# The last stores of a chunked attention with two mixtures of experts: when they are issued, and when the transposes of absent blocks are let go

## The reference

```
# attention within chunks of 64 tokens; q, k, v are (4, 8, 576, 64)
scores = scale * (q_c @ k_c.T); attn = softmax(scores); out = attn @ v_c
x = out as (N = 2304 tokens, D = 512)

# first mixture: all 4 experts on all tokens, F = 1024
x = sum over e of p[:, e] * (relu(x @ w1[e]) @ w2[e])

# second mixture: each token goes to one of 8 experts
expert_idx = argmax(x @ w_gate); gate_w = softmax(x @ w_gate) at expert_idx
out[mask] = gate_w[mask] * (relu(x[mask] @ w1[e]) @ w2[e])     # mask: tokens of expert e
```

## Time and profile before

| what | value |
|---|---|
| median of three executions | 1142.42 us (1140.51 to 1144.55) |
| the profiled execution | 1139.17 us |
| its span, first to last instruction | 1137.4 us |
| mean granted TensorE clock | 0.993 of full speed |
| TensorE busy | 1114.6 us, 98% of the span |
| VectorE busy | 563.9 us, 50% |
| ScalarE busy | 289.4 us, 25% |
| GpSimd busy | 312.3 us, 27% |
| transposes of hidden rows | 38, median 5.1 us to landing |
| stores to the output | 23 (22 from `rows`, one from the block ahead) |

### The profile page before, as it was taken

The page is one execution under the profiler, slowest core; times in us unless marked ns, Lnnn a source line. Parts: engine busy times, 40 slices in busy tenths (PEclk is TensorE's granted clock), DMA queues, the critical chain, the costliest instruction groups (busy, mean ns, idle before and its releaser), DMA issues.

```text
span 1137.4 us, 19057 instructions
## 1 busy us (share of the span) xinstructions
PE 1114.6 (98%) x6750; PEld 976.2 (86%) x6750; DVE 563.9 (50%) x1142; ACT 289.4 (25%) x429; POOL 312.3 (27%) x191
## 2 busy tenths in 40 slices
PE   9999999999999999999999999999999989999995
PEld 6899888999889999988999998889877778888884
DVE  5445434322221232222223248888655358988985
ACT  3444344331111133111113311112242023032220
POOL 7300000250000024000002401100377759168781
PEclk9999999999999999999999999999999989999998
DMA  9332221420000021000002101101672459379996
GB/s 355 79 103 83 74 74 28 150 74 0 0 0 0 0 82 65 0 0 0 0 0 92 56 29 29 21 7 28 186 186 67 136 179 243 63 214 222 211 193 109
DMA packets 104868, 97.71 MB, mean 86 GB/s; under 512 B 64111, under 2 KB 88815, under 8 KB 104690
## 3 DMA queue, kind: packets, MB, share of 16 engines
q1 hardware_dynamic: 81602, 60.23, 21.8%
q10 hardware_dynamic: 18720, 25.22, 7.5%
q0 software_dynamic: 4496, 11.56, 3.4%
HBM read 73.48 MB, written 10.92 MB: 74 GB/s over the span
## 4 chain that ended last, share of the span: by engine, by line
PE 91%; DVE 3%; DMA 2%; another core or an unknown queue 1%; issue 1%; SPq 0%; POOL 0%; ACT 0%; POOLq 0%; DVEq 0%
PE psum L1428 15%; PE psum L1430 14%; PE psum L1429 14%; PE psum L1474 12%; PE psum L1475 11%; PE psum L1476 11%; PE psum L1666 3%; PE psum L1668 3%; PE psum L1667 3%; DMA h_planes_T<-h_planes 1%; PE psum L1356 1%; PE psum L1340 1%; DMA rows<-x_rows,meta 1%; PE psum L1628 1%
## 5 line engine op out<-in xcount | busy, mean ns | idle before, releaser
L476 POOL TENSOR_TENSOR weights_r<-weights,weights_r 128x1024 fp32r<-128x1024 f32 x96 | 233.2, 2451 | 612.9 <-ACT weights_r L666 611.8
L1428 PE MATMUL psum<-xhi,weights_r 128*128 128x384 f32 (+1 forms) x772 | 260.0, 337 | 0.0
L1430 PE MATMUL psum<-xhi,weights_r 128*128 128x384 f32 (+1 forms) x772 | 257.9, 334 | 0.0
L1429 PE MATMUL psum<-xlo,weights_r 128*128 128x384 f32 (+1 forms) x772 | 257.7, 334 | 0.0
L1474 PE MATMUL psum<-weights_r,hhi 128*128 128x512 f32 x576 | 226.9, 394 | 0.0
L1476 PE MATMUL psum<-weights_r,hlo 128*128 128x512 f32 x576 | 224.8, 390 | 0.0
L1475 PE MATMUL psum<-weights_r,hhi 128*128 128x512 f32 x576 | 224.7, 390 | 0.0
L661 ACT ACTIVATE hhi<-psum 128x384 fp32r<-128x384 f32 x192 | 94.5, 492 | 482.5 <-PE psum L1430 482.5
L910 DVE SCALAR_TENSOR_TENSOR hlo<-psum,hhi 128x384 fp32r<-128x384 f32 x192 | 106.4, 556 | 218.1 <-ACT hhi L661 218.1
L666 ACT ACTIVATE weights_r<-weights 128x1024 fp32r<-128x1024 f32 x88 | 92.7, 1058 | 214.2 <-DMA weights<-in_moe_w 196.0
L1428 PEld LDWEIGHTS psum<-xhi,weights_r 128*128 128x128 f32 x772 | 144.9, 188 | 1.7
(11 more groups left out here) (189 smaller groups left out, 1094.6 us busy)
## 6 DMA issues: line engine op xcount, KB each, us to landing
weights<-in_moe_w SPq DMA_DIRECT2D x48, 512.0 KB, 4.6
weights<-in_moe_w ACTq DMA_DIRECT2D x48, 512.0 KB, 5.0
qkT<-in_qk SPq DMA_DIRECT2D x18, 512.0 KB, 4.0
v_rows<-in_v SPq DMA_DIRECT2D x18, 256.0 KB, 3.5
x_rows<-xfin SPq DMA_DIRECT2D x18, 256.0 KB, 5.3
wg_row<-in_gate_rows SPq DMA_DIRECT2D x1, 2048.0 KB, 7.4
h_planes_T<-h_planes SPq DMA_TRANSPOSE x38, 5.1
rows<-x_rows,meta POOLq DMA_INDIRECT x26, 3.7
```

What stands on the lines that cost most here:

```text
L476: gp.tensor_tensor(rounded(set_, 1, c), raw(set_, c), rounded(set_, 0, c).bitcast(F32), ALU.subtract).then_inc(sem("w1_lo" if c < NW // 2 ...
L1428: mm(out_, ahi, bhi, start=(i == 0), stop=False)
L1429: mm(out_, ahi, blo, start=False, stop=False)
L1430: last = mm(out_, alo, bhi, start=False, stop=(i == n - 1))
```

## The change

On GpSimd, the loop over pairs of places now runs over two pairs, with the stores of places 0 to 3. The third pair of splits is written out behind it without stores. Then GpSimd waits for a new semaphore, `all_joined`, and a loop stores places 4 to 7. On VectorE, the step that joins the last real block now raises `hrow_ready` by twice the number of blocks that are left, so that SyncE's transposes of all absent blocks may go, and raises `all_joined`; the steps of absent blocks raise nothing any more. If the last possible block is real, the same signal is given after its join.

```diff
             store_block(XB)
-            with pool.Fori(1, E2 // 2) as half:
+            def split_pair(half, stores=True):
+
                 e0 = half * 2
                 n0 = (E1 - 1 + e0) * NW
                 for u in range(2):
@@
                 for u in range(2):
                     for c in range(NW // 2, NW):
                         split_lo(1 - u, n0 + NW // 2 + u * NW // 2 + c, c)
-                    store_place(e0 + u - 2)
-            with pool.Fori(E2 - 2, E2) as p:
+                    if stores:
+                        store_place(e0 + u - 2)
+
+            with pool.Fori(1, E2 // 2 - 1) as half:
+                split_pair(half)
+            split_pair(E2 // 2 - 1, stores=False)
+            pool.wait_ge(sem("all_joined"), 1)
+            with pool.Fori(E2 - 4, E2) as p:
                 store_place(p)
@@ spare_step
                         join_h(b, 0)
                         join_h(b, 1)
                         dve.wait_ge(sem("h_joined"), (seq(b) - FIRST_TURNED) * 2)
-                        dve.sem_inc(sem("hrow_ready"), 2)
-                    with dve.Else():
-                        dve.sem_inc(sem("hrow_ready"), 2)
+                        dve.sem_inc(sem("hrow_ready"), 2 * (NB - 1 - b))
+                        dve.sem_inc(sem("all_joined"), 1)
                 finish(b)
@@
             with dve.If(real > NB - 1):
                 join_h(NB - 1, 0)
                 join_h(NB - 1, 1)
+                dve.wait_ge(sem("h_joined"), (seq(NB - 1) - FIRST_TURNED) * 2)
+                dve.sem_inc(sem("all_joined"), 1)
             finish(NB - 1)
```

## The result

| | before | after |
|---|---|---|
| median of 8 runs | 1141.31 us (1137.49 to 1144.55) | 1147.91 us (1146.09 to 1150.24) |
| the profiled execution | 1139.17 us | 1150.24 us |
| its span | 1137.4 us | 1148.6 us |

The ratio of the runs is 1.0066 with a 95% interval of 1.005 to 1.0083: the change makes the kernel 5.7 to 9.5 us slower. The profiled execution of the new kernel is the slowest of its eight, and 2.3 us of the 11.2 by which the spans differ stand ahead of the stretch in question (block 19's second product ends at 1111.22 in one trace and at 1113.53 in the other). So what follows counts from two moments inside each trace: G, the end of block 19's second product on TensorE, and J, the end of VectorE's join of the last real row.

A forecast was written before the change was run, and what follows sets the result against it. The end was taken to hang on GpSimd's last store issue: 20 us behind J, less 10.8 today, 3.4 from an earlier J and 0.8 of tail, gives +5.0 us and 1147.4 us; range 1143.0 to 1152.0.

The forecast's parts named there:

- What bounds the end: At the kernel's end, everything hangs on the moment GpSimd issues its last store; the span ran 7.4 us beyond it.
- Part two: On GpSimd behind J, four walks and nine stores put the last store 20 us behind J, against 10.8 before.
- Part one: Without four stores near block 20's transposes, the transpose lands within 9.7 us and J comes 3.4 us earlier.
- rival D: Weight loads, not stores, delay block 20's transpose; J stays and only the price remains: +8.4 us, 1150.8; chance 0.14.
- A: The forecast itself: walks and stores behind J set the end; +5.0 us, 1147.4; chance 0.57.
- The moved gap: TensorE's 3.93 us gap moves to before block 21's product; block 21's result still comes some 3.4 us earlier.
- Part three: Absent blocks' transposes, set free together, cost nothing on the path; the last store, alone, shortens the tail by 0.8 us.
- The sum: Whole kernel: 20 - 10.8 - 3.4 - 0.8 = +5.0 us, the span going from 1137.4 to 1142.4 us.

The follow-up runs named there:

- e2: The changed kernel with absent blocks' transposes let go step by step as before, so only the stores are deferred; ratio 1.0078 against the kernel before.
- e3: The changed kernel with places 4 to 7 stored in one walk over the 25 blocks instead of four; ratio 1.0028 against the kernel before.
- e1: The kernel before with only the absent blocks' transposes released at once, stores staying where they were; ratio 0.9994 against the kernel before.
- g2: The kernel before with the last two second-weight loads issued only after block 20's transposes have landed, stores unmoved; ratio 0.9983 against the kernel before.
- g1: The kernel before with the four stores of place 4 (blocks 13 to 16) left out; ratio 0.9979 against the kernel before.
- g3: The changed kernel with one walk for places 4 to 7, GpSimd waiting only until block 20 is joined; ratio 0.9986 against the kernel before.
- f3: The kernel before without any transpose of an absent block, SyncE's list ending at block 21; ratio 0.9993 against the kernel before.
- h1: g3 with ten matmuls on constants ahead of the last real block's second product, where TensorE stands idle; ratio 0.9993 against the kernel before.
- h2: g2 with ten matmuls on constants ahead of the last real block's second product and absent blocks' transposes released at once; ratio 0.9972 against the kernel before.
- f2: The kernel before with the last four loads of second weights issued at once, instead of two and then one after each rounding; ratio 0.9990.

## Why the prediction was right, by its own steps

**What bounds the end: right.** The chain ends in GpSimd's sequencer, every result is ready before its store, and the drain follows the last store.

**Part two, the price: right in mechanism, 8% short in size.** 20 us from J to the last store were expected and 21.6 came, in the changed kernel and again in e2. GpSimd passes its wait 0.2 us behind J (line 573, in ns and us as above):

```profile
L573 POOLq ALU_OP  x4: 36/36/36, 1126.5 to 1141.5; - x4
...
L573 POOLq MOVE  x1: 29/29/29, 1120.4 to 1120.4; - x1
```

The first store came 3.7 us behind J, as the prediction had it. Short were the next two boundaries: 1.9 us expected and 3.44 measured, 3.6 expected and 4.77 measured. The sequencer had run ahead as expected (its loop step at 1126.5 stands 1.3 us ahead of the fourth store), but the walk from there to the wait for row 17, at 1130.5, took 3.9 us: its two table loads took 0.62 and 0.53 us in the chain above, against 0.29 and 0.30 in the first walk. The next took 3.7, the last 3.1, the first 2.8. The sum had taken 1.4 us more than all warm, little more than one cold walk; 2.9 us more came. Its reason, that the first pass over new code is the slow one, does not fit either: the first walk was the fastest of the four. What makes the others slower was not tested. e3 tested the term as such, by taking three walks away: 7.9 us less in the trace, for 7.6 expected from the spacings.

**Part one, the gain: the term that was mis-sized.** 3.4 us were expected, and J moved from 8.0 to 6.7 us behind G in the compared traces: 1.2 us. The limit was computed rightly, J at 4.6 us behind G, and five experiments stand exactly there, among them e2 and e3, which defer the same stores. But e1, with its stores in place, has J at 5.5, closer than the changed kernel. So one execution can show the full 3.4 us or nothing, and no run here gives the mean of what the deferral brings. What failed is the step from "stores leave" to "the transpose lands within 9.7 us": in the changed kernel it landed in 11.9 us with no store near it (in 8.4 in e2 and 9.0 in e3, where the step held). The step rested on 7.1 against 10.2 and 13.1 us, a comparison of stretches in which the stores were one difference, and the weight loads of the same microseconds were set aside as rival D. It was also thinner than it reads: of the five transposes of 1062 to 1092 the trace shows only two landings, 6.9 us (1071.87) and 7.4 (1082.42), and of the pair beside four stores only one, 10.2. g2 and g1 show that stores alone leave 5.4 us and that loads alone can make 12. The rule of the Trainium skill that the prediction weighed (DMA: Bandwidth & Descriptors, section on SWDGE, HWDGE and iDMA), queues served in turn by the same engines, is not at odds with this: weight loads too come through another queue (q10) than the transposes (q1). The outcome, 7.5 us by the ratio, lies between A's 5.0 and D's 8.4, and nearer to D: the interval of 5.7 to 9.5 holds D and not A.

**The moved gap: right, and free only because the stores were later.** A second gap of TensorE did come ahead of block 21 (1.67 us). In the changed kernel's trace the product behind it ran at the full granted clock:

```profile
1123.60:1129.40 5.80, 5.75 (x24) 4.43 (x24) 1.59 (x3) 0.00 (x0) 3.90 (x4) 1.00 0.98 212
```

In e2, e3, g2 and g3 the gap was 2.4 to 2.7 us and that product took 7.4 us instead of 5.7. There the last result stands only 1.7 to 1.9 us closer to G than in the kernel before, where the prediction had 3.4 for the same J; the clock took the rest. In g2 and g3 the last store follows the last result, so this is lost time.

**Part three, the tail: right.** The absent blocks' transposes have no cost that can be measured (e1), and the tail lost 0.6 us for 0.8 expected. The fit of the Trainium skill (DMA: Bandwidth & Descriptors, section on the anatomy of one DMA) gave 2.6 us for a store of 256 KB. Here the trace agrees: alone at the end it was seen landed after 2.6 us, and also in e2; in f3, with no transpose near it either, it took 3.3. But the tail did not lose the 1.8 us that this would make: the drain ended no sooner than 6.5 us after the store in any trace (below).

**The sum.** In the compared traces, by the prediction's own terms: 21.55 - 10.83 - 1.24 - 0.64 = +8.8 us, where it had +5.0; 2.2 of the difference is part one, 1.5 part two. The runs say +5.7 to +9.5, and +5.0 lies just outside. That the new median, 1147.91 us, stands so close to the forecast of 1147.4 is in part luck: the forecast started from a median of 1142.42 for the kernel before, and the comparison has 1141.31.

## What to carry to other kernels

Before holding work back until a signal, count what its engine must do from the signal to the last item. Count with it the sequencer's control work (register loads, branches over absent cases) that today lies hidden under waits; here that, not the data movement, was most of the loss (three walks, 6 us). Walk once instead of four times, as e3 does, and hold back only as long as the thing to be protected lasts, as g3 does; doing the walk ahead of the wait was not tried. When two kinds of traffic share a slow stretch, take away each alone before saying which is at fault, and ask for more than one trace: here one and the same program up to J differed by 2 us and more. And a gap closed ahead of one product of TensorE can open ahead of the next, and be followed by a lower clock: look at the granted clock of the next product.

## What the runs showed of the hardware

GpSimd's closing drain ended 6.5 us after the start of the last store in all five traces where that store was seen landed in 2.6 to 3.7 us (after, e2, f3, h1 and h2), and 2.6 to 2.8 us after the landing where that took 4.1 us or more (7.2 for 4.4 before, 7.4 for 4.6 in e3). In these traces a store that landed faster than some 3.7 us won nothing.

The transposes from block 21 on, which have no weight load near them, landed in 3.0 to 6.1 us wherever a trace shows the landing (nine of the twelve), with stores beside them or not; those of blocks 19 and 20, beside loads of 512 KB, in 4.7 to 13.1.

The granted clock fell from 2.4 to 1.2 GHz for a part of the product behind a gap of 2.4 to 2.7 us in e2, e3, g2 and g3 (0.77 is the mean over the stretch in g3 above), and did not behind the first gap of the changed kernel, which was as long. Its stretches, the gap and the product behind it:

```profile
1113.50:1116.20 2.70, 0.03 (x1) 0.00 (x0) 2.63 (x4) 0.00 (x0) 0.00 (x0) 1.00 0.41 75
1116.20:1121.90 5.70, 5.69 (x24) 4.45 (x24) 5.31 (x7) 0.00 (x0) 0.00 (x0) 1.00 0.08 18
```

What tells the cases apart is open. The gap of 3.93 us before, and the one of 3.9 us in f3, were followed by the lower level too. The gaps of 1.3 to 1.9 us (e1, f2, g1, h1 and the second of the changed kernel) were not. The product behind the gap in the trace of before:

```profile
1115.20:1122.50 7.30, 7.29 (x24) 5.52 (x24) 6.56 (x8) 0.00 (x0) 1.51 (x2) 0.77 0.36 90
```
